# Attention and two expert layers on one core: probability tiles transposed by row halves, interleaved with the transpositions of keys, queries and leftover probabilities

## What is computed

```python
q_pool = q.reshape(B, H, S // factor, factor, D).mean(axis=3)
scores = scale * np.matmul(q_pool, k.transpose(0, 1, 3, 2))
scores = scores - np.max(scores, axis=-1, keepdims=True)
attn = np.exp(scores)
attn = attn / (np.sum(attn, axis=-1, keepdims=True) + 1e-09)
return np.matmul(attn, v).astype(np.float32)
```

## Time and profile before

| | us |
|---|---|
| median of 3 runs | 1127.43 |
| lowest, highest | 1125.4, 1127.88 |
| profiled execution, its own time | 1129.12 |
| its span, first to last instruction | 1127.4 |

### The profile page before, as it was taken

The page is one execution under the profiler, slowest core; times in us unless marked ns, Lnnn a source line. Parts: engine busy times, 40 slices in busy tenths (PEclk is TensorE's granted clock), DMA queues, the critical chain, the costliest instruction groups (busy, mean ns, idle before and its releaser), DMA issues.

```text
span 1127.4 us, 20403 instructions
## 1 busy us (share of the span) xinstructions
PE 1088.0 (97%) x6647; PEld 767.4 (68%) x6647; DVE 750.0 (67%) x1632; ACT 612.9 (54%) x1327; POOL 381.5 (34%) x454
## 2 busy tenths in 40 slices
PE   7899999999999999999899999997989999999996
PEld 4565665556656565655588888886768888888885
DVE  4777787777778777777548999898775633333110
ACT  5676666667666666665465434435356534343221
POOL 4545544454554445445322211215112211111101
PEclk8899999999999999999899999999999999999998
DMA  4221122212112221102520000004556653311100
GB/s 129 64 60 36 53 64 64 62 47 56 44 48 65 64 64 46 40 21 77 150 85 19 28 20 19 28 30 185 171 180 239 228 182 113 106 38 49 39 21 1
DMA packets 92705, 85.59 MB, mean 76 GB/s; under 512 B 49006, under 2 KB 69486, under 8 KB 92464
## 3 DMA queue, kind: packets, MB, share of 16 engines
q1 hardware_dynamic: 88592, 72.92, 21.0%
q0 software_dynamic: 4000, 11.28, 3.1%
HBM read 74.73 MB, written 11.27 MB: 76 GB/s over the span
## 4 chain that ended last, share of the span: by engine, by line
PE 44%; DVE 2%; issue 2%; POOL 1%; ACT 1%; DMA 1%; DVEq 0%; ACTq 0%; POOLq 0%
PE h_ps L694 8%; PE h_ps L696 8%; PE h_ps L695 8%; PE o_ps L694 5%; PE o_ps L696 5%; PE o_ps L695 5%; PE t_ps L1170 2%; PE t_ps L1062 1%; PE h_ps L1137 1%; PE h_ps L1186 1%; DVE junk L1266 1%; DMA w_raw_e<-in_moe_w 1%; DVE w_split L1480 0%; POOL x_lo L973 0%; PE h_ps L1084 0%
## 5 line engine op out<-in xcount | busy, mean ns | idle before, releaser
L346 POOL TENSOR_SCALAR probs<-probs,scales 128x576 f32<-128x576 f32 x288 | 209.8, 748 | 263.6 <-DVE scales L547 263.6
L642 ACT ACTIVATE probs<-s_ps,lows 128x576 f32<-128x576 f32 x288 | 211.0, 737 | 146.5 <-DVE lows L518 146.1
L518 DVE TENSOR_REDUCE lows<-s_ps 128x1 f32<-128x576 f32 x288 | 205.2, 753 | 59.1 <-PE s_ps L423 51.3
L371 PEld LDWEIGHTS t_ps<-ident,probs 128*128 128x128 f32 x1152 | 123.8, 141 | 108.4 <-issue 100.4
L423 PE MATMUL s_ps<-kt,qt 64*128 64x288 f32 x1024 | 163.9, 438 | 4.8 <-ACT probs L642 4.8
L371 PE MATMUL t_ps<-ident,probs 128*128 128x128 f32 x1152 | 158.8, 281 | 2.8 <-POOL probs L346 2.0
L472 PE MATMUL pv_ps<-pt,values 128*64 128x512 f32 x576 | 155.2, 618 | 1.0 <-DVE x_t L582 1.0
L556 DVE COPY pt<-t_ps 128x512 f32<-128x512 f32 x144 | 99.4, 690 | 43.7 <-PE t_ps L371 43.6
L423 PEld LDWEIGHTS s_ps<-kt,qt 64*128 64x128 f32 x1024 | 89.3, 190 | 43.4 <-issue 24.5
L992 POOL DMA_INDIRECT out<-junk,target_rows x25 | 29.5, 1182 | 261.0 <-ACT junk L1699 260.7
L637 ACT COPY pt<-t_ps 128x512 f32<-128x512 f32 x144 | 84.4, 586 | 28.5 <-PE t_ps L371 24.5
(11 more groups left out here) (257 smaller groups left out, 2056.2 us busy)
## 6 DMA issues: line engine op xcount, KB each, us to landing
w_raw_e<-in_moe_w SPq DMA_DIRECT2D x60, 512.0 KB, 5.5
k_raw<-in_k SPq DMA_DIRECT2D x32, 256.0 KB, 2.8
q_raw<-in_q SPq DMA_DIRECT2D x32, 256.0 KB, 3.2
token_rows<-x_rows SPq DMA_DIRECT2D x18, 256.0 KB, 2.0
values<-in_v SPq DMA_DIRECT2D x32, 128.0 KB, 2.7
values<-in_v SPq DMA_DIRECT2D x64, 64.0 KB, 2.7
w_raw<-in_moe_w_in SPq DMA_DIRECT2D x4, 512.0 KB, 5.0
w_raw<-in_moe_w_out SPq DMA_DIRECT2D x4, 512.0 KB, 3.8
```

The source lines that it names most:

```text
L346: nc.gpsimd.tensor_scalar(where, where, scales[:, g % 2, s, c:c + 1], 1.0, ALU.mult, ALU.mult).then_inc(norm_done if c else half_scaled, 1)
L371: last = nc.tensor.transpose(bank[:, i * P:(i + 1) * P], source, ident[:])
L518: nc.vector.tensor_reduce(lows[:, g % 2, s, c:c + 1], s_ps[c][:, :, 0:part], AX.XY, ALU.max, negate=True).then_inc(low_done[c], 1)
L642: nc.scalar.activation(two_halves(probs[g % 2][:, s, :])[:, :, columns(c)], s_ps[c][:, :, 0:part], ACT.Exp, bias=lows[:, g % 2, s, c:c + 1 ...
```

## The change

- **Turns by halves** (`turn_phase`, L469): each 128x128 transposition becomes two of 64 rows by 64 moving columns (rows 0 to 63 and 64 to 127 of the source). The lower half goes to `t_ps0`, the upper to `t_ps1`, so that each bank holds 64 queries of every tile; `pt`, the values' operand and the copy to `x_t` are laid out for that.
- **One phase with the third bank**: the third bank's transpositions are halved too and interleaved with the turns. The lower halves of the third bank come first beside upper halves of the turns, and the upper halves last. All waits of both, the one for the free third bank among them, stand ahead of the phase. From the second pair on, slots 0, 1, 2 and 7 hold KA, Q, TAILS and KB, slots 4, 5 and 6 the rest.
- **Queries** of both heads are transposed together (piece Q), copied to `qx`, and moved by four DMAs of SP to both row halves of `qt` (L271). QA and QB as pieces are gone (pair 0 apart).
- **Copies change engines and places**: `next_kq` is now DVE's, behind both `lowest` of the slot and the merges; `copy_rest` is now ACT's, behind both exponentials of the slot.
- **One slot later**: turning starts 11 slots behind the scores, not 10, and the probability tiles stand in a ring of 19.
- **Scales**: GpSimd forms the totals (L381, L385), DVE adds 1e-9 and inverts (`invert_totals`), GpSimd multiplies by two factors per tile.
- **Around it**: keys and queries of the second pair are turned in slots 4 to 7 of the first; empty transpositions (`warm`) are added in the first pair, at the end of the attention and at the start of the dense layer; four weight chunks load one pair earlier, and their high halves are made by DVE; the dense layer's first low half is made by DVE, not GpSimd.

```diff
-    kq_slots = {0: KA, 1: QA, 2: TAILS, 6: KB, 7: QB}
-    rest_slots = (3, 4, 5)
+    kq_slots = {0: KA, 1: Q, 2: TAILS, 7: KB}
+    first_kq_slots = {4: KA, 5: Q, 6: TAILS, 7: KB}
+    rest_slots = (4, 5, 6)
+    lag = slots + 2
+    ring = 2 * slots + 1
...
+            def move_queries(n):
+                sp.wait_ge(kq_out, kq_count(n, Q))
+                for h in range(2):
+                    first = h * (full + 1)
+                    for u in range(2):
+                        sp.dma_start(qt[n % 2][rows(u), first:first + full, :].rearrange("p t n -> p (t n)"),
+                                     qx[rows(h), :]).then_inc(q_moved, 16)
...
             for at in range(pairs + 1):
+                n = at + 2
+                if n < pairs:
+                    sp.wait_ge(kq_done, kq_count(n - 1, KA))
+                    load_a(n)
+                if at + 1 < pairs:
+                    move_queries(at + 1)
                 if at < pairs:
                     if at >= 2:
                         sp.wait_ge(pv_done, key_tiles * (at - 1))
                     load_values(at)
...
+            def turn_half(out, source, u):
+
+                return nc.tensor.transpose(out, source[rows(u), :], ident[rows(u), rows(u)])
+
+            def turn_phase(i, thirds, third_done):
+
+                pair, j = i // key_tiles, i % key_tiles
+                if j == 0:
+                    pe.wait_ge(norm_done, slots * (pair + 1))
+                if i > 0:
+                    pe.wait_ge(t_out[0], i)
+                    pe.wait_ge(t_out[1], i)
...
+                count = len(thirds)
+                for n in range(len(tiles) + count):
+                    if n < count:
+                        low_third = third_half(n, 0)
+                        if n == count - 1:
+                            low_third.then_inc(low_thirds, 1)
+                            low_third_count[0] += 1
+                    else:
+                        low_half = tile_half(n - count, 0)
+                    if n < len(tiles):
+                        high_half = tile_half(n, 1)
+                        if n == len(tiles) - 1:
+                            high_half.then_inc(t_done[1], 1)
+                    else:
+                        if n == len(tiles):
+                            pe.wait_ge(low_thirds, low_third_count[0])
+                        high_third = third_half(n - len(tiles), 1)
...
-                    if i is not None:
-                        turn_tiles(i, 0)
-                        turn_tiles(i, 1)
-                    third_visit(at, s, at)
-                    if at < pairs:
+                    thirds, third_done = third_blocks(at, s, at)
+                    if i is not None:
+                        turn_phase(i, thirds, third_done)
...
+            warm(s_ps[0][:, 0, :], 8)
...
+            def next_kq(g, s):
+
+                piece, par = kq_piece(g, s), 1 - g % 2
+                dve.wait_ge(kq_done, kq_count(g + 1, piece))
+                if piece == Q and g > 0:
+                    dve.wait_ge(q_moved, 64 * g)
```

More of the change, by code:

```diff
@@ L304, in _ @@
                     load_b(n)
[L305 to L307 removed]
+                if at == pairs - 2:
                     for c in range(stages):
@@ L340, in normalise @@
             def normalise(g, b):
-                pool.wait_ge(scales_ready, len(batches) * g + b + 1)
-                for s in range(*batches[b]):
+                par, (first, end) = g % 2, batches[b]
+                steps = 2 * (len(batches) * g + b)
+                pool.wait_ge(raises_done, len(batches) * g + b + 1)
+                pool.sem_inc(passed, 1)
+                nc.gpsimd.tensor_tensor(weighted[:, par, first:end, :], raises[:, par, first:end, :],
+                                        sums[:, par, first:end, :], ALU.mult).then_inc(total_steps, 1)
@@ L343, in normalise @@
+                pool.wait_ge(total_steps, steps + 1)
+                pool.sem_inc(passed, 1)
+                nc.gpsimd.tensor_tensor(total[:, par, first:end], weighted[:, par, first:end, 0],
+                                        weighted[:, par, first:end, 1], ALU.add).then_inc(total_steps, 1)
+                pool.wait_ge(recips_done, len(batches) * g + b + 1)
+                for s in range(first, end):
                     for c in range(2):
                         pool.sem_inc(passed, 1)
-                        where = two_halves(probs[g % 2][:, s, :])[:, :, columns(c)]
```

329 lines of the change are left out of this document (176 added, 153 removed).

## The result

| | before | after |
|---|---|---|
| median | 1127.46 us | 1158.49 us |
| lowest, highest | 1125.4, 1127.88 | 1155.35, 1160.79 |
| span of the profiled execution | 1127.4 | 1156.0 |

The ratio of after to before is 1.0277, 95% interval 1.025 to 1.0304: slower by 31 us. The forecast was 1168 (1132 to 1222), slower with a chance of 0.81.

The account below looks back on a forecast made before the run. The prediction took the order of work on TensorE, busy for 97%, as the bound. Start +2, 14 pairs +45, run-out -2 and seam -4 gave +41 on 1127.4: 1168 us, range 1132 to 1222.

Parts of the forecast that it names:

- What bounds after: TensorE busy near 75% in the attention, its waits before turns put down to copies at L637, L713 and L742.
- The step of halves: On TensorE, a step of halved turns takes 0.057 us (bounds 0.055 and 0.109, the latter today's).
- The rounds: Nine times a pair, from one slot's scores to the next: sum 36.0 us, 3.2 more than 32.79 before.
- Slot 3 to 4: DVE is late from slot 2, so slot 3's maximum starts at 2.02 us: a round of 3.69 us.
- Slot 8 to 0: Late maxima, inverse, merges of 0.93, then the x_t copy and 12 steps: a round of 5.82 us.
- 14 pairs: From slot 2 of the second pair on, 14 pairs each 3.24 us longer: +45 us (bounds +31 and +66).
- The start: Up to slot 2 of the second pair, DVE waiting in slot 8 until about 36: +2 us (-3 to +6).
- The run-out: Last pair and run-out: no keys in slot 7, weights early, but one slot more: -2 us (-5 to +4).
- The seam: Attention to dense layer: about 1 us less wait and 3 for the clock, -4 us (bounds -5 and 0).
- hidden, faster: Rival: third bank free whenever TensorE comes to it, pairs of 26.1 or about 27 us, about 1042 us; chance 0.14.
- The load sets the step: Rival: halved turns on TensorE still take 0.109 us a step, +3.5 us a pair, about 1217 us; chance 0.12.
- The clock falls: Rival: TensorE at its lower clock level in slots 4 to 6, half of the pairs, +46, about 1214 us; chance 0.12.

Follow-up runs that it names:

- rest: The changed kernel with ACT's three copies of the rest directly behind its turned copy, ahead of both exponentials: 1111.53 us, ratio 0.9868.
- both: As rest, with DVE's copies of keys and queries also ahead of both maxima from the second pair on: 1081.0 us, ratio 0.9597.
- full: The changed kernel with each turn and third-bank block one whole transposition of 128 columns again: 1236.54 us, ratio 1.098.
- rest+g: As rest, with GpSimd adding later queries and tails between batch 1's totals and scaling, from the second pair on: 1092.69 us, ratio 0.9692.

## Why the prediction was right, point by point

- **What bounds after**: right. In the window of a whole pair, 60 to 94.5 us, TensorE is busy for 27.44 of 34.50 (granted clock 1.00), and what it waits for are the copies of lines 637, 713 and 742. "rest" shows it for 713 with nothing but ACT's copies moved, "both" for 637. The forecast busy share was 75%, it is 80%.
- **The step of halves**: taken as 0.057, measured 0.062 (pairs of halves at 220.56, 220.62, 220.68). The fixed 0.15 between turns and scores is gone, as taken. From 227.09 to 227.63 eight steps take 0.54 with the hand-over. "full" gives what it is all worth: 5.6 us a pair.
- **The rounds**: 36.0 predicted, 34.52 measured. Six of the nine are within 0.11 of the forecast, 5 to 6 is off by 0.22, and two terms were mis-sized. Slot 3 to 4: 3.24 for 3.69; the small operations and copies of DVE overlap in the rows, and the forecast had added them end to end. Slot 8 to 0: 4.99 for 5.82. There I put the merges beside a busy GpSimd, 0.93; they took 0.35 (rows below), and the round ended with ACT's exponentials, not with DVE:

```profile
249.86 0.16 DVE L614 TENSOR_TENSOR low<-lows 128x1 f32<-128x1 f32 x1
250.05 0.16 DVE L617 TENSOR_TENSOR below<-low,lows 128x2 f32<-128x2 f32 x1
...
250.48 0.20 ACT L753 ACTIVATE raises<-below 128x2 f32<-128x2 f32 x1
250.58 0.21 ACT L742 COPY x_t<-third_ps 128x64 f32<-128x64 f32 x1
```

  In the earlier trace rows the same merges took 0.24 and 0.69, while GpSimd was scaling; after, it is not, since it waits for DVE's inverse of this batch until 250.16.
- **14 pairs**: +45 predicted, +26.7 measured (slot 2 of the second pair at 50.07, of the last at 534.87, against 44.39 and 502.51 before). The nine rounds were 1.5 too long, 14 x 1.5 = 21; two long last rounds, 1.7 each, give 3 of it back.
- **The start**: +2 predicted (-3 to +6), +5.7 measured. The mechanism was the one named, the third pair's loads behind moves and values, with GpSimd's total behind them; DVE waited until 38.55, not 36.
- **The run-out**: -2 predicted, 0.0 measured (from slot 2 of the last pair to the start of the last values 48.24 before, 48.25 after). This term was mis-sized: nothing was gained there.
- **The seam**: -4 predicted, -3.8 measured; 1 of the forecast was for the wait and 3 for the clock. From the first product to the end it is 568.22 for 570.98, so 2.8 for the clock (in the kernel before the first twelve products take 5.29 us to the start of the thirteenth, after 2.9, which is 2.4 of it); from the last values' start to the first product it is 4.66 for 5.67 (583.12 to 587.78), so 1.0 for the wait. The sizes were right, one reason was not: I took the empty transpositions as what keeps the clock. Without them it stays up as well, and with GpSimd's low half too. Either the shorter wait or the empty transpositions suffices; the run without both was not made.
- **Sum**: 5.7 + 26.7 + 0.0 - 3.8 = 28.6, the difference of the spans. Predicted was 41. That the forecast came within 10 us is in part luck: the start was 3.7 worse and the run-out 2 worse than forecast, which hides some of the 18 us by which the pairs were better.
- **The rivals**: "hidden, faster" needed each of six rounds about half a microsecond shorter (the waits of 9.9 less the 3.2 by which a pair got longer are 6.7, not the 6.9 of the prediction); only one of the six was, 8 to 0 by 0.83. "The load sets the step" fell with the measured 0.062: the Trainium skill, "TensorE: Matmul & The Clock Gate", section "LDWEIGHTS (loading the stationary operand)", gives columns divided by 1.2 ns whatever the rows, which makes 107 ns for 128 columns, an estimate. As a bound on the step the trace does not bear it out: two loads in different row halves go into each step of 62 ns. "The clock falls" did not happen in the pairs, though TensorE was busy for only 27.4 of 34.5 us. It did in the fill, where TensorE waited 12.05 us: from 31 to 60 us the granted clock is 0.71. The windows of the kernel after (busy time and instructions of PE, PEld, DVE, ACT and POOL, granted clock, DMA):

```profile
60.00:94.50 34.50, 27.44 (x342) 15.27 (x342) 23.56 (x49) 20.56 (x54) 17.50 (x28) 1.00 0.25 59
31.00:60.00 29.00, 14.09 (x118) 8.04 (x116) 12.23 (x27) 10.26 (x28) 10.97 (x19) 0.71 0.37 97
```

## What to carry to other kernels

When a wait is moved ahead of other work, look first at what releases it: here the same phase stood in a kernel 31 us slower than before with the releasing copies at the end of their engine's slot, and in one 72 us faster with them at the front, where ACT was idle anyway. The second kernel has two smaller changes besides, GpSimd's order and the third pair's queries first; moving ACT's three copies alone was worth 47 us. Halving transpositions by rows pays in full only if the neighbours on TensorE have the same shape; each change of shape took back about 0.15 us. And when the slots get shorter, read the chain again: the next links were GpSimd's order and one copy in slot 3, neither of them visible at first.

## What the hardware showed that I had not expected

DVE's small `below` (L617, two operands in SBUF) takes 0.16 us, but in two pairs of the kernel after it took 2.33, and the round behind it grew from 4.99 to 6.67. Timeline of the first:

```profile
174.79 1.65 POOL L392 TENSOR_SCALAR probs<-probs,raises,recips 128x576 f32<-128x576 f32 x2
175.77 2.33 DVE L617 TENSOR_TENSOR below<-low,lows 128x4 f32<-128x4 f32 x1
176.41 1.26 POOL L363 TENSOR_TENSOR q_sum<-q_raw 128x512 f32<-128x512 f32 x1
177.63 0.46 POOL L373 TENSOR_TENSOR tail_sum<-q_tail 128x128 f32<-128x128 f32 x1
```

It ends with GpSimd's third instruction in a row (177.63 + 0.46 = 178.09). In another pair it took 0.61 (246.53 to 247.14) and ended with the scaling alone. The maxima and copies from PSUM beside the same GpSimd instructions keep their 1.41 and 0.68. The Trainium skill, "SBUF — State Buffer", section "SBUF: two separate sides", says that a DVE instruction with two SBUF inputs and a GpSimd instruction that reads SBUF exclude each other, and that the one that comes later is blocked for the whole instruction; the rows agree, and show more: a row of GpSimd instructions without a gap can hold DVE through all of them. It need not: in "rest", `low` and `below` (0.71 and 0.77, shown above) each ended within the same row of four scalings, one behind the other. With the queries added elsewhere (rest+g) no `below` lasts over 0.682, and no pair of that profile has the long last round. But the same holds for the run with the third pair's queries first (0.741 at most, every pair of the steady part 34.5 to 34.6), where GpSimd's order is that of the change, so the order alone does not bring the long ones about. What decides whether DVE gets in between two of GpSimd's instructions stays open.

GpSimd's scaling of a half tile by two factors takes 824 ns, by one factor before 748 (mean of one on the pages of after and of before). What this alone costs was not tested.
